# Merging two attention bursts of a fused RWKV-attention and two-MLP kernel, with the work around them reordered

## The reference

```python
# attention: r, k, v are [4, 8, 768, 48]; w, u are [8, 48]
for t in range(S):
    cur = einsum('bhd,bhe->bhde', u * kt, vt)
    y[:, :, t] = einsum('bhd,bhde->bhe', rt, state + cur)
    state = w * state + einsum('bhd,bhe->bhde', kt, vt)
# first MLP: x is y as [3072, 384]; w1, w2 [384, 1024]; w3 [1024, 1024]; w_out [1024, 384]
y2 = ((x @ w1) * (x @ w2) @ w3) @ w_out
# second MLP: w_in [384, 2048], w_out [2048, 384]
h = y2 @ w_in
out = (h * cos(h)) @ w_out
```

## Time and profile before

| | |
|---|---|
| median of 3 runs | 799.14 us (798.84 to 799.3) |
| the profiled execution, its own time | 798.6 us |
| its span, first to last instruction | 797.1 us |
| TensorE busy | 790.3 us (99%), 6716 matmuls |
| VectorE busy | 426.9 us (54%) |
| ScalarE busy | 380.5 us (48%) |
| GpSimd busy | 353.6 us (44%) |

### The profile page before, as it was taken

The page is one execution under the profiler, slowest core; times in us unless marked ns, Lnnn a source line. Parts: engine busy times, 40 slices in busy tenths (PEclk is TensorE's granted clock), DMA queues, the critical chain, the costliest instruction groups (busy, mean ns, idle before and its releaser), DMA issues.

```text
span 797.1 us, 16246 instructions
## 1 busy us (share of the span) xinstructions
PE 790.3 (99%) x6716; PEld 708.1 (89%) x6716; DVE 426.9 (54%) x648; ACT 380.5 (48%) x663; POOL 353.6 (44%) x289
## 2 busy tenths in 40 slices
PE   8999999999999999999999999999999999999997
PEld 5999999999999999999988888888888888888886
DVE  7977545344444454323379555545555554554553
ACT  4633322222222222233467667656665665665664
POOL 5546746464645647422224444334333432432432
PEclk9999999999999999999999999999999999999999
DMA  8773524232424234122222010001001001001001
GB/s 333 253 241 98 153 77 153 62 114 77 134 76 138 93 98 133 31 73 68 80 80 60 0 41 1 1 0 40 1 0 40 1 0 41 1 0 38 3 0 40
DMA packets 47598, 57.36 MB, mean 72 GB/s; under 512 B 21794, under 2 KB 34211, under 8 KB 47523
## 3 DMA queue, kind: packets, MB, share of 16 engines
q1 hardware_dynamic: 34898, 45.56, 18.0%
q10 hardware_dynamic: 12624, 10.75, 4.4%
HBM read 46.86 MB, written 9.44 MB: 71 GB/s over the span
## 4 chain that ended last, share of the span: by engine, by line
PE 92%; DVE 2%; POOL 2%; DMA 2%; issue 1%; ACT 0%; ACTq 0%; POOLq 0%; DVEq 0%; SPq 0%
PE p_h L1123 25%; PE p_acc L1123 12%; PE p_a L1123 12%; PE p_b L1123 12%; PE p_out L1323 8%; PE p_out L1322 8%; PE p_out L1326 8%; PE p_s L1132 1%; PE p_acc L1257 1%; PE p_y L1144 1%; PE p_y L1148 1%; PE p_kv L1136 1%; DVE w3t_l L944 1%; DVE state L899 1%; DMA w_raw<-in_moe_w3t 1%
## 5 line engine op out<-in xcount | busy, mean ns | idle before, releaser
L613 POOL TENSOR_TENSOR g_l<-g,g_h 128x512 fp32r<-128x512 f32 x96 | 149.9, 1562 | 240.9 <-ACT g_h L799 240.9
L477 POOL TENSOR_TENSOR g_l<-g,g_h 128x384 fp32r<-128x384 f32 x64 | 73.6, 1150 | 116.9 <-ACT g_h L647 116.9
L1072 DVE TENSOR_TENSOR g<-angle,p_h 128x512 f32<-128x512 f32 x96 | 65.8, 686 | 109.2 <-ACT angle L808 109.2
L1123 PE MATMUL p_h<-y_h,wi_h 128*128 128x512 f32 x288 | 112.1, 389 | 0.0
L1123 PE MATMUL p_h<-y_l,wi_h 128*128 128x512 f32 x288 | 112.1, 389 | 0.0
L1322 PE MATMUL p_out<-g_h,wq_l 128*128 128x512 f32 x288 | 112.0, 389 | 0.0
L1323 PE MATMUL p_out<-g_h,wq_h 128*128 128x512 f32 x288 | 112.0, 389 | 0.0
L1123 PE MATMUL p_h<-y_h,wi_l 128*128 128x512 f32 x288 | 112.0, 389 | 0.0
L799 ACT CAST g_h<-g 128x512 fp32r<-128x512 f32 x96 | 59.6, 621 | 67.2 <-PE p_out L1326 42.4
L647 ACT CAST g_h<-g 128x384 fp32r<-128x384 f32 x64 | 32.9, 514 | 114.2 <-DVE g L928 114.2
L804 ACT ACTIVATE angle<-angle 128x512 f32<-128x512 f32 x96 | 60.6, 631 | 49.7 <-DVE angle L1082 49.7
(11 more groups left out here) (110 smaller groups left out, 1690.1 us busy)
## 6 DMA issues: line engine op xcount, KB each, us to landing
krT_raw<-in_kr_dims SPq DMA_DIRECT2D x24, 512.0 KB, 4.2
kr_raw<-in_kr_tokens SPq DMA_DIRECT2D x24, 384.0 KB, 4.6
v_raw<-in_v_tokens SPq DMA_DIRECT2D x24, 192.0 KB, 2.6
x_raw<-y_transposed SPq DMA_DIRECT2D x24, 192.0 KB, 2.5
out<-out_sb SPq DMA_DIRECT2D x18, 256.0 KB, 2.2
stage_b<-in_moe_w_in SPq DMA_DIRECT2D x8, 384.0 KB, 3.1
stage_b<-in_moe_w_out SPq DMA_DIRECT2D x8, 384.0 KB, 3.0
w_raw<-in_moe_w3t ACTq DMA_DIRECT2D x5, 512.0 KB, 5.7
```

Source lines behind the costliest of these rows:

```text
L477: nc.gpsimd.tensor_tensor(g1_l[:, n % 2, :], g1[:, n % 2, :], g1_h[:, n % 2, :].bitcast(F32), ALU.subtract).then_inc(s_gl, 1)
L613: nc.gpsimd.tensor_tensor(g2_l[:, par, :], g2[:, par, :], g2_h[:, par, :].bitcast(F32), ALU.subtract).then_inc(s_g2l, 1)
L1072: nc.vector.tensor_tensor(g2[:, n % 2, :], angle[:, n % 2, :], p_h[n % 4][:, :], ALU.mult).then_inc(s_g2, 1)
L1123: ins = mm(dst, lhs(x), rhs(y), start=first and q == 0 and p == 0, stop=last and q == len(tiles) - 1 and p == 2)
```

## The change

- Burst (None, 2) and burst (3, None) become one burst (3, 2), at tile f = 5 after t = 6 (it was t = 2). Step 0 has three bursts, (4, 3), (5, 4), (6, 5), in slots 0, 2 and 4, like the other steps. VectorE's `scale_k_dims(3)`, `scale_r_dims(3)`, `sum_kur(3)`, `take_sums(3)` and GpSimd's `decay_first(4)` move into the prologue, and SP loads chunk 4's keys and chunk 3's values earlier.
- The low parts of pieces 0 and 1 of w_out are made by VectorE, not by GpSimd; k_pairs is made after the check of w's range; GpSimd waits for the first `w3t_low` before `scale_k(1)`.
- Piece 0 is loaded by SP, as its first DMA, not by ScalarE. ScalarE splits piece 3 before it copies k_table.
- In the last slot of all, the two high matmuls of the last tile come after the low ones of the others, and the last store is issued by ScalarE.

```diff
-    bursts = {0: (3, None), 1: (4, 3), 3: (5, 4), 4: (6, 5)}
-    for j in range(1, NSTEP - 1):
+    bursts, k_at, raw_at, scaled_at, z_at = {}, {}, {}, {}, {0: HC + 1}
+    for j in range(NSTEP - 1):
         for i in range(HC):
-            n = HC * (j + 1) + i
-            bursts[NF * j + 2 * i] = (n + 1 if n + 1 < NCH else None, n)
-    scaled_at, raw_at, k_at, z_at = {2: 5, 3: 6, 5: 7}, {1: 5, 3: 6, 5: 7}, {1: 5, 2: 6, 5: 7}, {0: 4, 3: 5, 4: 6, 6: 7}
...
+            n, slot = HC * (j + 1) + i, NF * j + 2 * i
+            bursts[slot] = (n + 1 if n + 1 < NCH else None, n)
+            if n + 2 < NCH:
+                k_at[slot], raw_at[slot + 1], scaled_at[slot + 1], z_at[slot + 2] = n + 2, n + 2, n + 2, n + 2
...
# SP
+        sp.dma_start(A_SLOTS[0], wo_st[0].rearrange("p j c -> p (j c)")).then_inc(s_st[0], 16)
         sp.dma_start(w_col[:, :, 0], w_dims).then_inc(s_w, 16)
...
         load_v(2)
         turn_over(0)
+        load_krT(4)
+        load_kr(4)
+        load_v(3)
         turn_over(1)
         turn_over(2)
-        load_v(3)
-        load_krT(4)
-        load_kr(4)
...
# GpSimd
-        for i in POOL_PIECES:
-            piece_low(i)
...
+        pool.wait_ge(s_wtl, 1)
         scale_k(1)
...
         times_r(4)
+        decay_first(4)
         low(0)
...
# ScalarE
-        start_piece(0)
...
-        for i in range(3):
+        for i in range(NWO):
             piece(i)
         act.wait_ge(s_tabT, 1)
         nc.scalar.copy(k_table[:, :, :], ...)
-        piece(3)
...
+        act.wait_ge(s_oa, copied_act(NG - 1, KT - 1))
+        act.dma_start(out[(KT - 1) * P:KT * P, (NG - 1) * G:NG * G], out_sb[:, KT - 1, :]).then_inc(s_out, 16)
...
# VectorE: the copies to k_pairs now stand here, behind the range check
+        piece(0)
+        piece(1)
+        piece(2)
         scale_k_dims(0)
         scale_r_dims(0)
-        piece(2)
         piece(3)
...
         w34_low(3)
+        scale_k_dims(3)
         w3t_low(5)
         take_sums(2)
+        scale_r_dims(3)
         piece(4)
         x_low(0, 0, 0)
         w34_low(4)
         w3t_low(6)
         piece(5)
-        scale_k_dims(3)
-        scale_r_dims(3)
+        sum_kur(3)
         x_low(0, 0, 1)
         w34_low(5)
         w3t_low(7)
-        sum_kur(3)
+        take_sums(3)
+        scale_k_dims(4)
+        scale_r_dims(4)
         w34_low(6)
         x_low(0, 0, 2)
-        scale_k_dims(4)
-        scale_r_dims(4)
         w34_low(7)
...
# TensorE
-                elif (f, t) == (5, 2):
-                    burst(None, 2)
+                elif (f, t) == (5, 6):
+                    burst(3, 2)
...
             for t in range(KT - 1):
                 if f == 0:
                     bank_free(t)
                 by_high(t)
             if n < NF2 * NG - 1:
                 if f == 0:
                     bank_free(KT - 1)
                 by_high(KT - 1)
             pe.wait_ge(s_g2l, n + 1)
             for t in range(KT):
                 if n == NF2 * NG - 1 and t == KT - 1:
                     by_high(t)
                 ins = by_low(t)
```

More of the change, by code:

```diff
@@ L307, in copied_dve @@
         return g + 1
[L309 to L315, removed]
     def diagonal_done(n):
         return (s_diag0, n + 1) if n < HC else (s_diag, n + 1 - HC)
-    bursts = {0: (3, None), 1: (4, 3), 3: (5, 4), 4: (6, 5)}
-    for j in range(1, NSTEP - 1):
+    bursts, k_at, raw_at, scaled_at, z_at = {}, {}, {}, {}, {0: HC + 1}
+    for j in range(NSTEP - 1):
         for i in range(HC):
-            n = HC * (j + 1) + i
-            bursts[NF * j + 2 * i] = (n + 1 if n + 1 < NCH else None, n)
-    scaled_at, raw_at, k_at, z_at = {2: 5, 3: 6, 5: 7}, {1: 5, 3: 6, 5: 7}, {1: 5, 2: 6, 5: 7}, {0: 4, 3: 5, 4: 6, 6: 7}
-    for slot, (n, _) in bursts.items():
-        if slot >= NF and n is not None and n + 1 < NCH:
-            k_at[slot], raw_at[slot + 1], scaled_at[slot + 1], z_at[slot + 2] = n + 1, n + 1, n + 1, n + 1
+            n, slot = HC * (j + 1) + i, NF * j + 2 * i
+            bursts[slot] = (n + 1 if n + 1 < NCH else None, n)
+            if n + 2 < NCH:
+                k_at[slot], raw_at[slot + 1], scaled_at[slot + 1], z_at[slot + 2] = n + 2, n + 2, n + 2, n + 2
     piece_at = {0: NWO + 4, 1: NWO + 5, 2: NWO + 6, 3: NWO + 7}
@@ L415, in _ @@
             for t in range(KT):
+                if (g, t) == (NG - 1, KT - 1):
+                    break
                 if t == 1:
@@ L656, in start_piece @@
             if i >= 4:
-                act.wait_ge(*low_done(i - 4))
+                act.wait_ge(s_stl, i - 3)
                 act.wait_ge(s_w34, WHOLE)
@@ L759, in step @@
                     if slot == X_SLOTS[0]:
-                        act.wait_ge(*low_done(NWO + 6))
+                        act.wait_ge(s_stl, NWO + 7)
                     x_high(j + 1, (j + 1) % 2, X_SLOTS.index(f))
@@ L969, in _ @@
         assert steps[0] == CHAIN
[L970 to L973, removed]
         dve.wait_ge(s_row, 16)
@@ L982, in _ @@
         nc.vector.tensor_tensor(by_token[:, :], w_range[:, 2:3], w_range[:, 3:4], ALU.add).then_inc(s_checked, 1)
+        for q in range(2):
+            nc.vector.tensor_copy(
+                k_pairs[half[q], :, :, :],
+                powers[half[q], q::2, 0:SUB].unsqueeze(2).broadcast_to([HEAD, HP, 2, SUB])).then_inc(s_pairs, 1)
+        piece(0)
+        piece(1)
+        piece(2)
         scale_k_dims(0)
         scale_r_dims(0)
-        piece(2)
         piece(3)
@@ L1278, in _ @@
         burst(0, None)
-        for i in range(NWO):
-            pe.wait_ge(*low_done(i))
+        pe.wait_ge(s_stl, NWO)
         for f in range(WHOLE, NF):
@@ L1305, in project, with bank_free @@
         def project(g, f):
+            def bank_free(t):
+                g_old, t_old = divmod(KT * g + t - NOUT, KT)
+                if g_old < 0:
+                    pe.wait_ge(s_y2, NSTEP + 1)
+                elif t_old == 1:
+                    pe.wait_ge(s_od, copied_dve(g_old, t_old))
+                else:
+                    pe.wait_ge(s_oa, copied_act(g_old, t_old))
             n = NF2 * g + f
@@ L1311, in project, with by_high, by_low @@
                 pe.wait_ge(s_bl, NWI + f // 2 + 1)
-            for t in range(KT):
+            def by_high(t):
                 cols = slice(t * P, (t + 1) * P)
[L1314 to L1321, removed]
                 mm(bank[t][:, :], wq_l[:, f, cols], g2_h[:, f % 2, :], start=f == 0, stop=False)
                 mm(bank[t][:, :], wq_h[:, f, cols], g2_h[:, f % 2, :], start=False, stop=False)
-            pe.wait_ge(s_g2l, n + 1)
-            for t in range(KT):
+            def by_low(t):
                 ins = mm(bank[t][:, :], wq_h[:, f, t * P:(t + 1) * P], g2_l[:, f % 2, :], start=False, stop=f == NF2 - 1)
@@ L1328, in project @@
                     ins.then_inc(s_o, 1)
+                return ins
+            for t in range(KT - 1):
+                if f == 0:
+                    bank_free(t)
+                by_high(t)
+            if n < NF2 * NG - 1:
+                if f == 0:
+                    bank_free(KT - 1)
+                by_high(KT - 1)
+            pe.wait_ge(s_g2l, n + 1)
+            for t in range(KT):
+                if n == NF2 * NG - 1 and t == KT - 1:
+                    by_high(t)
+                ins = by_low(t)
             ins.then_inc(s_used, 1)
```

13 lines of the change are left out of this document (4 added, 9 removed).

## The result

The changed kernel takes 800.34 us (median of 20 executions, 799.79 to 802.86); the kernel before, run beside it, 798.97 (20 executions, 798.37 to 799.79). The ratio over all executions is 1.0021, interval 1.0014 to 1.0028, that of the two medians 1.0017: 1.4 us slower, right at the bound of 0.2% that the prediction had drawn. The forecast was 799.4. Six of the changed kernel's 20 executions took 801.48 or more, three of them with a mean granted clock of 1.0; no trace shows why.

What follows compares the result with a forecast made beforehand. TensorE, 99% busy, bounds the kernel, with VectorE equally loaded in the prologue. Step 0's start +3.1, its burst -2.2, step 1's wait -0.3, end -0.3: +0.3 on 798.6, plus 0.5 to the median, 799.4 us; range 796.3 to 801.0.

Steps and rivals of the forecast that it cites:

- The merge on TensorE: Step 0 loses a burst of 2.2 us, the one in tile 5 grows by 0.1: net -2.1 us on TensorE.
- rival D: Bursts: merging saves nothing because the fuller burst takes the sum of both halves; 801.6 us, chance 0.02.
- The end: Last slot: store issued from ScalarE's queue -0.35 us, low matmuls behind GpSimd's last g_l +0.05; together -0.3.
- Leg 1: Prologue from first w3t_l (18.08 to 19.29): tile 2 gains 0.4, lost again by burst (1, 0), at 27.2 as before.
- rival C: Start: w_col lands late behind 384 KB on SP, delaying TensorE's transposes; landing at 8 gives 800.7 us; chance 0.04.
- Leg 2: Prologue up to rT_sc(2): +0.5 us stays in VectorE's queue, so burst (2, 1) starts at 34.07, not 33.58.
- Leg 3: Prologue up to w3t_l(6): added scaling and sums on VectorE make tile 6 start at 45.5 instead of 43.95, +1.5 us.
- the strict taking of turns: VectorE and GpSimd under the exclusive lock: overlapping instructions end one behind the other, each waiting until the other is through.
- Rival B: Prologue stalls are larger, each further collision or late tokens 0.9 us; step 0 at +4.9 gives 801.2; chance 0.09.
- DMAs don't decide here: Prologue loads: chunk 4's keys asked for at about 34.5, chunk 3's values at 36, ahead of uses at 48 and 41.5.
- Leg 4: Prologue up to step 0: x_l(2) ends at 55.4, TensorE waits 1.6 us, step 0 starts at 55.5, +3.1.
- the forecast's own case: Step 0 starts 2 to 4 us later than before; 798.2 to 800.4 us, chance 0.55.

Runs made afterwards that it cites:

- the end alone: Kernel before with only the last slot's new matmul order and the last store issued by ScalarE: 798.45 us against 798.98.
- w_col first: Changed kernel with the loads of w_col and w_row ahead of piece 0's on SP's queue, as before the change: 803.0 us against 798.98.
- the merge alone: Kernel before with the merged burst, the new VectorE and SP orders and decay_first(4), without the start's and end's edits: 799.81 us against 798.65.
- the new order: VectorE makes w34_l(4), w3t_l(6) ahead of piece(4), w3t_l(7) ahead of piece(5); on the merge with early x_low(2) and faster end: 798.72 us against 799.07.
- all three edits: Changed kernel with w_col and w_row ahead of piece 0, x_low(2) ahead of chunk 4's scaling, chunk 3's values ahead of chunk 4's keys: 802.2 us against 798.65.

## Why the prediction was right, and where its sum was not

**The merge on TensorE: right.** From step 0's start to step 1's it is 42.62 us instead of 45.05, -2.43, where -2.2 for the burst and -0.3 for the wait ahead of step 1 were summed; the matmuls at 99.45 and 99.62 stand 0.17 apart, so that wait is gone; that kur(6) is what removed it, as forecast, wasn't tried. In the rows around step 0's first burst, 65.43 - 63.15 = 2.28, the same as the earlier trace rows: both halves cost what one does, and rival D is refuted.

**The end: right.** -0.44 against -0.3, shown by the trace of the end alone as well.

**Leg 1: mis-sized by 0.8 on VectorE, and read wrong by 0.4 on TensorE.** The first w3t_l did take 1.21, as predicted, and the second ended at 23.91, as predicted (23.96). But the first started at 19.10 and not at 18.08: the start "in both" behind ScalarE was wrong. The price of w_col's late landing had been set against TensorE's transposes only, and there it was nearly hidden: used at 6.20 where I had estimated 5.1, it cost a wait of 0.16 us at 11.53. VectorE's own queue had no such slack: behind the powers come k_pairs, four pieces, kT_sc, rT_sc and w3t_l. GpSimd, waiting for w3t_l, came 1.0 later too (k_sc to 21.41 instead of 20.35), and so kur fell behind the second w3t_l, and rT_sc(1) had to wait for kur, to 25.34. That is the 0.8 at the state. With w_col first, the first w3t_l ended 1.8 sooner and step 0 came 0.9 sooner; without GpSimd's wait, the state came 0.6 to 0.9 sooner. This is rival C's cause by a way that rival C didn't have. The 0.4: I let burst (1, 0) start 0.1 behind the state's end. Where TensorE does wait for the state, it starts 0.46 behind it: 27.86 to 28.32 in the changed kernel, 26.36 to 26.82 with w_col first, 26.79 to 27.25 in the merge alone. Before's 27.16, 0.55 behind the state, was no such wait: TensorE had worked without a gap up to it.

**Leg 2: right.** From the state to rT_sc(2), 6.88 us against 6.86.

**Leg 3: mis-sized by 0.75.** Up to rT_sc(3), at 41.47, only leg 1's 0.8 is missing. Then piece(4) was summed at 1.5 (decay, then piece) and took 2.5, since ku went ahead of it too; 0.2 came back behind it. The merge alone on the old start shows the same 2.56. The step that failed is the strict taking of turns, which the prediction read from one place; before's x_l at 39.78, ahead of the very ku and behind the very decay in question, already spoke against it. Rival B named a further collision of this kind, "each further collision 0.9", though at the second piece, piece(5), or at an x_l and not at piece(4), with a chance of 0.09; 4.61 at step 0 is beyond its point of +4.4, short of its +4.9.

**"DMAs don't decide here": wrong as a statement, right in the sum.** Chunk 3's values came 1.0 late for burst (3, 2). I had them asked for at 36, and so they were, about, but the issue on SP's queue alone took 1.54 us, and they landed some 6 us after it, at 42.97:

```profile
36.98 1.54 SPq L351 DMA_DIRECT2D v_raw<-in_v_tokens  x1
```

Loading them first gained nothing, as VectorE was behind anyway; once it was not, the same microsecond was worth 0.7 to 0.9.

**Leg 4: right.** From w3t_l(6) to x_l(2) 9.91 us against 10.0, and a wait at step 0 of 1.57 against 1.6. Moving x_l(2) by one place in the queue took the whole wait away.

**The sum.** Leg 1's 0.8 and leg 3's 0.75 are the 1.5 us by which step 0 is later than forecast. In spans it is +1.7 instead of +0.3, in medians +1.4 instead of +0.3. That a change which takes 2.1 us off TensorE gains nothing came from the right place, VectorE's prologue; its size was 1.1 us too kind in medians, inside the forecast's range by a little (800.34 of 800.4), and that by luck: step 0 came later than the +2 to +4 of the forecast's own case, and the +0.5 from the profiled execution to the median was 0.04 (800.3 to 800.34). With the 0.5 added the same execution would have given 800.8, outside 800.4.

Shown by experiment: the wait at step 0 is x_l(2)'s place, the start's edits cost 0.7, the merge with its orders 1.2, and the end gives back 0.4 in the spans: together 1.5, where 1.4 was measured. Tile 6 is held by two things at once, w3t_l(6)'s place behind piece(4) and the late values: early values alone gave nothing (47.00 to 46.98), with the new order they gave 2.2 (44.80). On the old start the new order alone gave 0.3, both 1.85. Open: the long executions with w_col first, and with them what that order alone is worth as a median.

## What to carry to other kernels

Before work is moved into a stretch, write out the queue of the helper engine there, with what stands behind each moved piece and when TensorE needs it: the same merge cost 1.2 us with one order of VectorE's queue and, with the new end, gained 1.6 with another, which puts first what TensorE waits for first. Taking away one wait shows nothing while a second stands right behind it: the late values were worth 0 us behind the late w3t_l, and 0.7 to 0.9 once that was gone. A cost that is called hidden must be hidden on every engine that waits for it, not only on the one that sets the time. And a price for two engines in each other's way should be read at the very pair of instructions that the change will meet: the old trace had that pair, and its x_l of 2.17 us showed what a VectorE instruction pays there.

## What the runs showed of the hardware

- GpSimd kept the shared access over two instructions while a VectorE instruction that had been issued in between waited: the decay, 40.89 to 42.17, and ku, to 43.13, with piece(4) waiting from 41.39 to its end at 43.95. It came again in every run with piece(4) directly behind rT_sc(3) (2.55 to 2.57 us), and before with x_l at 39.78 (2.17). In the earlier trace rows the engines took turns, and they also did where GpSimd's two instructions followed each other without a gap: in the changed kernel w3t_l(7), issued at 49.41, ended at 50.73, between the diagonal (to 49.65) and k_sc(4) (49.61 to 51.60). In the cases where GpSimd kept it, the VectorE instruction had been issued while the decay itself still waited for VectorE. What decides wasn't tried.
- w_col, 4 KB, landed 4.6 us after its issue with 384 KB ahead of it in SP's queue (after), and 2.6 us (before) and 2.2 us (w_col first) after it with nothing ahead. This agrees with what the prediction took from the Trainium skill, DMA: Bandwidth & Descriptors, "Queues, rings and completion order": w_col landed at 6.10, behind piece 0 at 5.71.
- The same load of 384 KB, piece 0, issued at the same 1.88, landed at 5.85 in one execution and at 7.76 in another (w_col first, and all three edits).
- Behind 1.94 us of idling in the middle of the program the granted clock fell to 0.51, the level of 1.2 GHz, for 3.5 us, which cost about 1.5 us. In the changed kernel's own trace waits of 0.8 to 1.4 us, with small matmuls between them, brought no such stretch, and neither did 1.95 us at the same place in the profiled execution with the values loaded early (mean clock 0.999). Six of that kernel's other executions had 0.997 or 0.998; where their low stretches lay wasn't seen, and they were not longer.
